# Gated attention and two MLPs on one core: two heads in column halves of the array, compact values and states, seven w_out slots, another order of the front

## The reference

```python
for t in range(S):
    state = f[:, :, t, :, None] * state + np.einsum('bhd,bhe->bhde', k[:, :, t], v[:, :, t])
    y[:, :, t] = np.einsum('bhd,bhde->bhe', q[:, :, t], state)
```

## Time and profile before

| | us |
|---|---|
| runs of the kernel | 919.07, 920.27, 920.87 (median 920.27) |
| the profiled execution | 919.11 |
| its span, first to last instruction | 917.4 |
| front, to the first `up` | 61.7 |
| attention steps beside `up` | 61.7 to 358 |
| PE busy over the span | 857.0 (93%) |
| DVE, ACT, POOL busy | 486.3, 373.7, 227.9 |

### The profile page before, as it was taken

One profiled execution on the slowest core, in us unless ns is written; L12 is line 12 of the kernel. 1 busy time (PEld: TensorE's weight loads), 2 busy tenths in 40 slices (PEclk: granted clock), 3 DMA queues, 4 the chain that ended last, 5 costly groups with the idle time before them and its releaser, 6 DMA issues.

```text
span 917.4 us, 16237 instructions
## 1 busy us (share of the span) xinstructions
PE 857.0 (93%) x6097; PEld 769.5 (84%) x6097; DVE 486.3 (53%) x1269; ACT 373.7 (41%) x826; POOL 227.9 (25%) x226
## 2 busy tenths in 40 slices
PE   4769999999999999999999999999877999999994
PEld 3548888888888888888888888889777999999994
DVE  7347656666666653546677877777612222222120
ACT  5345555445545543533223333322223444444431
POOL 5800000000001000120000000000015677777741
PEclk9879999999999999999999999999997999999998
DMA  9735444444455434554544543434402555555510
GB/s 232 209 81 140 119 136 138 130 121 136 133 139 137 130 100 146 195 189 121 150 138 127 155 128 116 129 90 128 155 36 81 161 169 148 165 159 184 166 50 26
DMA packets 80214, 123.66 MB, mean 135 GB/s; under 512 B 32912, under 2 KB 57488, under 8 KB 80144
## 3 DMA queue, kind: packets, MB, share of 16 engines
q1 hardware_dynamic: 65488, 75.23, 30.1%
q0 software_dynamic: 10560, 42.48, 13.1%
q10 hardware_dynamic: 4096, 5.02, 2.3%
HBM read 83.37 MB, written 34.60 MB: 129 GB/s over the span
## 4 chain that ended last, share of the span: by engine, by line
PE 84%; DVE 10%; DMA 2%; issue 1%; ACT 1%; POOL 1%; SPq 0%; ACTq 0%; POOLq 0%; DVEq 0%
PE ps_h L1375 14%; PE ps_h L1377 13%; PE ps_h L1376 13%; PE ps_y L1348 5%; PE ps_heads L1321 4%; PE ps_heads L1375 4%; PE ps_heads L1376 3%; PE ps_heads L1377 3%; PE ps_gate L1417 3%; PE ps_k L1484 3%; PE ps_gate L1375 2%; PE ps_u L1375 2%; PE ps_k L1328 2%; PE ps_gate L1377 2%; PE ps_gate L1376 2%; PE ps_u L1377 2%
## 5 line engine op out<-in xcount | busy, mean ns | idle before, releaser
L1375 PE MATMUL ps_h<-x_hi,w_hi 128*128 128x384 f32 x576 | 206.3, 358 | 8.3 <-DVE x_lo L1041 7.1
L1377 PE MATMUL ps_h<-x_hi,w_lo 128*128 128x384 f32 x576 | 195.3, 339 | 0.0
L1376 PE MATMUL ps_h<-x_lo,w_hi 128*128 128x384 f32 x576 | 194.8, 338 | 0.0
L874 ACT ACTIVATE g_hi<-qk 128x384 fp32r<-128x384 f32 x128 | 67.1, 525 | 176.1 <-PE ps_h L1377 95.4
L1046 DVE TENSOR_TENSOR w_raw<-ps_h,w_raw 128x384 f32<-128x384 f32 x128 | 71.2, 556 | 122.3 <-ACT w_raw L845 121.9
L1375 PEld LDWEIGHTS ps_h<-x_hi,w_hi 128*128 128x128 f32 x576 | 109.7, 190 | 16.8 <-issue 8.5
L682 POOL DMA_DIRECT2D g_kept<-w_raw x64 | 34.8, 544 | 338.8 <-DVE w_raw L1046 338.8
L1376 PEld LDWEIGHTS ps_h<-x_lo,w_hi 128*128 128x128 f32 x576 | 110.0, 191 | 0.0
L1377 PEld LDWEIGHTS ps_h<-x_hi,w_lo 128*128 128x128 f32 x576 | 109.5, 190 | 0.0
L732 POOL TENSOR_TENSOR w_lo<-w_raw,w_hi 128x1536 fp32r<-128x1536 f32 x28 | 97.9, 3512 | 40.6 <-ACT w_hi L918 40.5
L845 ACT ACTIVATE w_raw<-ps_h 128x384 f32<-128x384 f32 x128 | 62.4, 488 | 95.7 <-PE ps_h L1377 95.4
(11 more groups left out here) (202 smaller groups left out, 1714.0 us busy)
## 6 DMA issues: line engine op xcount, KB each, us to landing
g_kept<-w_raw POOLq DMA_DIRECT2D x64, 384.0 KB, 2.9
qk<-g_kept SPq DMA_DIRECT2D x64, 384.0 KB, 3.3
w_raw<-w SPq DMA_DIRECT2D x32, 768.0 KB, 4.5
qk<-qkf SPq DMA_DIRECT2D x64, 144.0 KB, 3.4
vals<-v SPq DMA_DIRECT2D x64, 72.0 KB, 3.9
x_rows<-cum_rel POOLq DMA_DIRECT2D x24, 192.0 KB, 4.1
qk<-qkf SPq DMA_DIRECT2D x60, 72.0 KB, 2.2
w_raw<-w_in POOLq DMA_DIRECT2D x4, 768.0 KB, 7.7
```

Of the source, the lines that this page charges most:

```text
L874: nc.scalar.activation(g_hi[:, n % GB, :], g_raw[:, slot, n % 2 * BLK:(n % 2 + 1) * BLK], ACT.Copy)\
L1375: nc.tensor.matmul(to, a_hi, b_hi, start=start, stop=False)
L1376: nc.tensor.matmul(to, a_hi, b_lo, start=False, stop=False)
L1377: last = nc.tensor.matmul(to, a_lo, b_hi, start=False, stop=stop)
```

## The change

Values are kept 96 wide, without the zeros, and loaded with one DMA for each pair and block instead of two. The state of each head is 48 columns wide in its own 48 partitions, so the mask goes and L1014 becomes a multiplication with one scalar. The update, y and the state's part of y become two matmuls each, one for each head, whose 48 columns lie in column half 0 or 64 of the array; for the state the 48 rows lie in row half 0 or 64 too. y now stands in partitions 0 to 47 and 64 to 111, and `ship` sends each head by itself: 2, 3, 3 and 2 DMAs for the four pairs instead of 1, 2, 2 and 1. Two memsets of PSUM replace those of the mask and of the values.

In the front there are seven slots for w_out, and SP issues all 16 tiles before the gates, keys and values of block 1. Turn-outs begin at step 4, the last two and the last `gate_out` follow the last step. The gates of pairs 2 and 3 are worked one to two steps earlier. Behind the last step the cumulation of pair 4 comes ahead of the first split; `factors` and `scale` of pair 5 move behind `up` 0, and `turn_gates` behind `up` 1. Block 1's steps take slots 1 to 12, later blocks start one slot later. The first load of w_in waits for gates instead of keys.

```diff
@@ -45,7 +45,7 @@
 HP = 64 + HD
-PV = 3 * HD
+PV = 2 * HD
 PACE = 14
...
@@ -65,11 +65,11 @@
 GATE_LAG = 2
-WIN = 4
+WIN = 7
 OUT_SLOT = 102
-AHEAD = 2
+AHEAD = 1
 TURN_SLOTS = 5
-TURNS = {3: 1, 4: 1, 5: 2, 6: 2, 7: 2, 8: 2, 9: 2, 10: 2, 11: 2}
+TURNS = {4: 1, 5: 1, 6: 2, 7: 2, 8: 2, 9: 2, 10: 2, 11: 2}
 FIRST_PIECE = 40
...
@@ -101,8 +101,8 @@
         k_rows = sb("k_rows", [P, 2, HP])
-        state = sb("state", [HP, PAIRS, 2, 2 * HD])
-        state_sum = sb("state_sum", [HP, PAIRS, 2 * HD])
+        state = sb("state", [HP, PAIRS, 2, HD])
+        state_sum = sb("state_sum", [HP, PAIRS, HD])
         y_pair = sb("y_pair", [P, PAIRS, BLK])
...
@@ -197,8 +196,8 @@
         turn_row_banks = [ps_heads[:, 0, :], ps_k[:], ps_y[:]]
-        y_area = ps_y[0:2 * HD, 0:P]
-        update_area = ps_u[0:HP, 0:2 * HD]
+        y_area = ps_y[0:HP, 0:P]
+        update_area = ps_u[0:HP, 0:HD]
         key_area = ps_k[:, 0:HP]
...
@@ -357,8 +355,8 @@
                 yield "logs", m
-            beside = {1: [("cumulate", 2)], 2: [("factors", 2)], 3: [("cumulate", 3), ("scale", 2)],
-                      4: [("factors", 3)], 5: [("scale", 3)]}
+            beside = {0: [("cumulate", 2)], 1: [("factors", 2), ("cumulate", 3)], 2: [("scale", 2), ("factors", 3)],
+                      3: [("scale", 3)]}
             f = 0
...
@@ -372,19 +370,19 @@
             yield from settle(STEPS - 1)
+            while f < FT:
+                yield "turn_out", f
+                f += 1
+            yield "gate_out", FT // 4 - 1
             yield "logs", 4
+            yield "cumulate", 4
+            yield "split", 0, 0
+            yield "split", 0, 1
             yield "logs", 5
-            yield "gate_out", FT // 4 - 1
-            yield "turn_gates", 0
-            yield "split", 0, 0
-            yield "cumulate", 4
-            yield "split", 0, 1
             yield "cumulate", 5
+            yield "split", 0, 2
             yield "factors", 4
-            yield "split", 0, 2
             yield "scale", 4
-            yield "factors", 5
-            yield "scale", 5
...
@@ -393,7 +391,7 @@
                 t, i = divmod(n, STEPS)
-                at.setdefault(i if t == 1 else (t - 1) * PACE - AHEAD + i * PACE // STEPS, []).append(n)
+                at.setdefault(i + 1 if t == 1 else (t - 1) * PACE - AHEAD + i * PACE // STEPS, []).append(n)
             first = {n // (2 * CB): slot for slot, ns in at.items() for n in ns if n % (2 * CB) == 0}
...
@@ -407,6 +405,11 @@
                 yield "up", t, j
+                if slot == 0:
+                    yield "factors", 5
+                    yield "scale", 5
+                if slot == 1:
+                    yield "turn_gates", 0
                 if slot >= GATE_LAG and (slot - GATE_LAG) % 4 == 3:
...
@@ -541,10 +544,9 @@
                 t, hp = divmod(m, PAIRS)
-                vsrc = v[t // 2 * PAIRS + hp].rearrange("p (c h d) -> p c h d", c=CH, h=2)
-                vdst = vals[:, hp].rearrange("p c (h d) -> p c h d", d=HD)
-                for h in range(2):
-                    sp.dma_start(vdst[:, :, 2 * h], vsrc[:, t % 2 * CB:(t % 2 + 1) * CB, h]).then_inc(v_in[hp], 16)
+                at = t % 2 * CB * PV
+                sp.dma_start(vals[:, hp].rearrange("p c n -> p (c n)"), v[t // 2 * PAIRS + hp][:, at:at + CB * PV])\
+                    .then_inc(v_in[hp], 16)
...
@@ -559,22 +561,19 @@
                 load_keys(m)
+            for m in (2, 3):
+                load_values(m)
             sp.wait_ge(gate_w_zeroed, 1)
             sp.dma_start(gate_w[:, :, 0:EXPERTS], w_gate.rearrange("(k p) e -> p k e", p=P)).then_inc(gate_in, 16)
-            load_out_tile(0)
-            load_values(2)
-            load_out_tile(1)
-            load_values(3)
-            for f in range(2, WIN):
+            for f in range(FT):
                 load_out_tile(f)
-            for m in range(PAIRS, 2 * PAIRS):
-                load_gates(m)
-            for what, *a in opening():
-                if what == "turn_out" and a[0] + WIN < FT:
-                    load_out_tile(a[0] + WIN)
-                elif what == "ship":
-                    load_keys(PAIRS + a[1])
-                    load_values(PAIRS + a[1])
+            for group in (range(PAIRS, PAIRS + 2), range(PAIRS + 2, 2 * PAIRS)):
+                for m in group:
+                    load_gates(m)
+                for m in group:
+                    load_keys(m)
+                for m in group:
+                    load_values(m)
             for m in range(2 * PAIRS, 3 * PAIRS):
...
@@ -652,15 +650,17 @@
                 .then_inc(consts, 1)
-            pool.wait_ge(consts, 6)
+            pool.wait_ge(consts, 5)
             nc.gpsimd.memset(qk[32:64, 2:4, 0:2], 0.0).then_inc(zeroed[1], 1)
                 _, src, tiles = weight_piece(g, 0)
-                if g < 2:
-                    pool.wait_ge(qk_in[g], 32)
+                if g == 0:
+                    pool.wait_ge(f_in[1], 32)
+                if g == 1:
+                    pool.wait_ge(qk_in[1], 32)
...
@@ -808,24 +808,26 @@
                     reached(act, xt_in[hp], 16 * ship_parts(hp) * t)
-                nc.scalar.activation(y_pair[0:2 * HD, hp, cb * P:(cb + 1) * P], y_area, ACT.Copy)\
+                nc.scalar.activation(y_pair[0:HP, hp, cb * P:(cb + 1) * P], y_area, ACT.Copy)\
                     .then_inc(y_copied, 1)
             def ship_parts(hp):
-                return 1 if hp in (0, PAIRS - 1) else 2
+                return 2 if hp in (0, PAIRS - 1) else 3
                 reached(act, x_lo_ready, (t - 1) * KT)
-                row = hp * 2 * HD
-                done = 0
-                while done < 2 * HD:
-                    k, p = divmod(row + done, P)
-                    n = min(P - p, 2 * HD - done)
-                    act.dma_start(xT[p:p + n, t % 2, k, :], y_pair[done:done + n, hp, :]).then_inc(xt_in[hp], 16)
-                    done += n
+                for h in range(2):
+                    row = (2 * hp + h) * HD
+                    done = 0
+                    while done < HD:
+                        k, p = divmod(row + done, P)
+                        n = min(P - p, HD - done)
+                        act.dma_start(xT[p:p + n, t % 2, k, :], y_pair[64 * h + done:64 * h + done + n, hp, :])\
+                            .then_inc(xt_in[hp], 16)
+                        done += n
...
@@ -964,17 +966,15 @@
             nc.vector.memset(qk[32:64, 0:2, 0:2], 0.0).then_inc(zeroed[0], 1)
-            nc.vector.memset(pair_mask[:], 0.0).then_inc(mask_zeroed, 1)
-            dve.wait_ge(mask_zeroed, 1)
-            for h in range(2):
-                nc.vector.memset(pair_mask[64 * h:64 * h + HD, h * HD:(h + 1) * HD], 1.0).then_inc(consts, 1)
+            nc.vector.memset(ps_u[0:HP, 0:HD], 0.0).then_inc(consts, 1)
+            nc.vector.memset(ps_y[0:HP, 0:P], 0.0).then_inc(consts, 1)
                 if m == 0:
-                    dve.wait_ge(consts, 6)
+                    dve.wait_ge(consts, 5)
                 nc.vector.tensor_tensor_scan(cum, restart[:], log_f[0:HP, m % 2, :], 0.0, ALU.mult, ALU.add)\
...
@@ -1011,9 +1011,8 @@
                 c = t % 2 * CB + cb
-                nc.vector.scalar_tensor_tensor(out=state[:, hp, before % 2, :], in0=src,
-                                               scalar=step_f[:, hp, factor:factor + 1], in1=pair_mask[:],
-                                               op0=ALU.mult, op1=ALU.mult).then_inc(state_ready, 1)
+                nc.vector.tensor_scalar(state[:, hp, before % 2, :], src, step_f[:, hp, factor:factor + 1], None, ALU.mult)\
+                    .then_inc(state_ready, 1)
...
@@ -1331,26 +1330,29 @@
                 if cb == 0:
-                    pe.wait_ge(v_in[hp], 32 * (t + 1))
+                    pe.wait_ge(v_in[hp], 16 * (t + 1))
                 if has_keys(n):
                         pe.wait_ge(*update_read[kb - 1])
-                    both_heads = vals[:, hp, cb, :].rearrange("p (h d) -> p h d", d=HD)[:, 0:3:2, :]
-                    nc.tensor.matmul(update_area, k_rows[:, kb % 2, :], both_heads, start=True, stop=True)\
-                        .then_inc(update_done, 1)
+                    for h in range(2):
+                        last = nc.tensor.matmul(update_area[64 * h:64 * h + HD, :], k_rows[:, kb % 2, 64 * h:64 * h + HD],
+                                                vals[:, hp, cb, h * HD:(h + 1) * HD], start=True, stop=True)
+                    last.then_inc(update_done, 1)
                 pe.wait_ge(scores_masked, n + 1)
                 for h in range(2):
-                    last = nc.tensor.matmul(y_area, vals[:, hp, cb, h * HD:h * HD + 2 * HD],
-                                            scores[:, n % 2, h], start=h == 0, stop=c == 0 and h == 1)
+                    last = nc.tensor.matmul(y_area[64 * h:64 * h + HD, :], vals[:, hp, cb, h * HD:(h + 1) * HD],
```

(12 more changed lines are left out.)

## The result

The changed kernel takes 932.65 us (median of 4 runs, 932.5 to 932.71) against 919.67 us before (4 runs, 915.7 to 920.87): 1.0149 times as long, interval 1.0117 to 1.018, slower by 13 us. The forecast was 921.2 with a range to 931. The profiled execution has a span of 930.9 us (before 917.4).

A forecast was written before the change was run, and what follows sets the result against it. PE was taken to bound the kernel behind the front, and to wait only in the front. Front -10.0, steps +9.1, `turn_gates` +1.7 and block 1's x +0.7 sum to +1.5 us; forecast 921.2 us, range 911 to 931.

The forecast's parts named there:

- The step: Attention steps in slots: transpose to `up` streaming takes 1.13 to 1.14 us instead of 1.00; 84 steps cost +9.1 us.
- Rival C: Steps in slots: changes of array division cost less than those seen, say half; 909 us, faster; chance 0.13.
- B: Rival: the state's two half products write one PSUM bank and run one after the other; +15.7 us, 937; chance 0.10.
- `turn_gates`: Between `up` 1 and the first score: PE waits for `leak` and the copy, then turns the gates; +1.7 us.
- the ship's additional DMA: Slots: one more DMA, 32 times, 0.55 to 0.6 us of ACT each, hidden by PE's work; uncovered 18 us.
- +0.7 (0 to 2.5): Block 1's x: shipping one slot later and one DMA more, partly won back, cost 0.7 us.
- a wait of under 2.5 us before block 1: Sign to look for: PE waits less than 2.5 us before block 1's first `up`.
- the front's "-10.0": Front: `up` 0 starts at 52 us (51 to 53) instead of 61.72, 10.0 us gained; bounds -5 and -14.
- clock, worth 2: Front: fewer pauses on PE avoid time at the lower clock, gaining 2 us.
- w_out's wait: Front: 4.4 us of PE's idle time come from late w_out tiles and go with seven slots.
- if all goes well: Front: the last y's copy ends at 43.5 us in the good case, about 44.3 otherwise.
- less idle keeps the clock: Front: with less idle time on PE the clock stays up, worth 2 us.

The follow-up runs named there:

- e1: Kernel before with only the column halves, compact values and states, and per-head ships; old front, slots and four w_out slots: 930.29 us, ratio 1.0138.
- e3: Kernel before with the new front, whole-array matmuls and four w_out slots, attention steps in their old slots: 911.63 us, ratio 0.991.
- e4: Changed kernel with the later attention steps put back in their old slots: 925.05 us, ratio 1.0062.
- e5: e2 with only the ship of y changed, issued by head, 10 DMAs a block instead of 6: 918.62 us, ratio 1.0003.
- e14: Changed kernel with the gates' work of each block's last slot but one put behind the next slot's split of x: 930.59 us, ratio 1.0133.
- e6: Changed kernel with 20 matmuls of 128x128 zeros on PE ahead of the first score: 928.46 us, ratio 1.0117.
- e9: e6 with two more matmuls of zeros in each of the front's twelve steps: 938.88 us.
- e2: Kernel before with the new front and steps one slot later, but whole-array matmuls and four w_out slots: 911.23 us, ratio 0.9918.
- e8: Kernel before with halves for update and values, but the state as one block-diagonal 112x112 matmul ahead of the update; old front and slots: 929.42 us, ratio 1.0126.
- e13: e8 with the update too as one whole-array 112x96 matmul, masked on DVE, so only the values' matmuls stay in halves: 940.03 us, ratio 1.0225.
- e7: e3 with 20 matmuls of 128x128 zeros on PE ahead of the first score: 909.74 us, ratio 0.9908.
- e11: e7 with one more matmul of zeros in each of the front's twelve steps: 911.52 us.
- e10: Changed kernel with four w_out slots instead of seven: 932.43 us.
- e12: Changed kernel with the gates' work of pairs 8 and on started one slot earlier: 934.73 us.

## Why the prediction was wrong

**The step was right.** 1.15 us measured for 1.13 to 1.14, 0.095 at each change of division in the rows, y's pairs 0.007 us apart. e1's blocks are 9.3 us longer. Without the longer waits before blocks 3 and 6 (1.25), and with 2.0 us less at half clock in block 0 put back (1.0), that is 9.0 for 9.1 forecast. (The forecast's terms as written add up to 9.3; with 12 x 0.01 for its 0.2 they give 9.1.) Rival C is out. So is B, whose 937 is the rivals' number nearest to the 932.65 measured. The state's two products write one bank from different row halves and start 0.007 us apart, so what the Trainium skill says ("TensorEngine Tiling (Array Packing)", Gotcha 1: PSUM Pressure), that different row tiles can't access the same bank simultaneously, doesn't hold back this pair, whose partitions of the bank are disjoint too: all 80 such pairs of the trace start 0.006 or 0.007 us apart.

**`turn_gates` was right.** 1.1 us of wait (forecast 1.2), and block 0 in e3 is 1.1 longer than before with 1.3 us less of it at 1.2 GHz, so 1.8 for 1.7.

**The step that failed first: the ship's additional DMA "in slots ... is hidden by PE's own work", and "+0.7 (0 to 2.5)" for block 1.** It looked at the slack of one landing and at nothing else that stands in ACT's order ahead of x_hi. PE waits 2.31 us before block 1, 2.03 before block 3 and 0.51 before block 4, and no longer 0.53 before block 6: 4.0 more than before. Two waits inside blocks are new, 0.4 for scores in block 1 and 0.9 for `leaky` in block 4. Behind the two long waits 10.2 us run at half clock; e4's blocks 1 and 3, without a fall, are 1.5 and 3.0 us shorter once the waits are taken out, so 4.5 are lost. That is 9.8 where 0.7 stood. The sum behind `up` 0 then is 9.0 + 1.8 + 9.8, less 0.4 for less half clock in block 0: 20.2, measured 19.9. The prediction's own sign, a wait of under 2.5 us before block 1, came true; its price for that wait, and the clock behind it, did not.

e5 shows the cause of block 3's wait without any halves, e14 that ACT's queue makes half of it. Block 1's is a landing (x_hi waited 2.64 us for the transfer), and its cause is open: it was 2.06 to 2.46 us in the four kernels with halves and shift but no warm matmuls, 0.40 and 0.42 in the two with them (e6, e9), and 0.30 and 0.41 in e2 and e5.

**The step that failed second: the front's "-10.0", of it "clock, worth 2".** w_out's wait went, as forecast, and PE's idle time between first step and last y fell from 7.8 to 0.7 us, more than the 6 forecast. But the last y ended at 46.6 instead of 44, because the rise of the clock moved from 19 to 36 us: 24.5 us of the steps run at 1.2 GHz, 15.1 before. The tail behind took 8.9 for 8.5. The prediction's own terms give less than its 10.0, too: 44.3 and 8.5 are 52.8, 8.9 before 61.72, and even the 43.5 of "if all goes well" gives 9.7. The new front by itself gave 9.2 (e3) and 12.2 (e2), so the forecast of it was right for whole-array matmuls. It was the halves, and what goes with them, that spent it: e4's `up` 0 is 6.8 later than e3's and the changed kernel's 6.1 later than e2's, while 12 steps at 0.14 are 1.7. The prediction took "less idle keeps the clock" for granted; the changed front has less idle and less clock.

**Why the sum missed.** Both failures are meetings of two parts: e1 adds 10.5, e3 takes 8.1, sum +2.4, near the forecast of +1.5; together (e4) they are +5.3; with the shift, which alone costs nothing, +13. The last step, 7.6 us, is clear of the noise. The 2.9 between +2.4 and +5.3 is not: e1 and e3 alone are known to 3 us each. There only the start of `up` 0 speaks for a meeting. The range held none of this, as it added independent bounds. Its chances are off by a little as well: the parts named for "slower" add up to 0.44, not 0.42.

**What stays open.** Why the clock rises later with the halves. More work doesn't bring the rise forward (e9), leaving out the state's halves doesn't either (e8, 33.2), and e13 lies between. The ships by head alone don't do it (e5, 22.5), but compact values beside whole matmuls were not tried. A kernel with halves in the slots only was not tried; neither was one in which block 1's landing is made early. And nothing here shows why the long matmuls of e8 and e13 are slower.

**The better version.** The new front with whole-array matmuls and four slots: e2, e3, e7 and e11 are 909.7 to 911.6 us, 0.991 to 0.992 of before, and faster than the changed kernel by 21 to 23 us. Warm matmuls add nothing that can be told from e3.

## What to carry to other kernels

Halving the columns of short matmuls buys streaming time and pays a gap of 0.095 us at every change of division, and the first weights in the open: count the changes before the columns. When each PE stage begins with an operand from an in-order engine, list all that its queue issues in the slot ahead, DMA issues included, and price a new wait with the clock that may fall behind it. Two edits that are each harmless may meet in one slot: time them alone and together.

## What was not expected of the hardware

- With column halves in its steps, a TensorE that was busy for 23.2 of 24.0 us (11 to 35 us) stayed at its lower speed, while before, busy for 19.9 of the same 24.0, it rose at 19 us. Whole-array matmuls put between (e9) made the slow time longer.
- Waits of 1.0 to 1.6 us before block 3 left the clock alone six times (e1, e2, e4, e8, e13, e14); each of 2.03 to 2.46 before blocks 1 and 3 (the changed kernel, e5, e6, e9, e10, e12, e14) came with 3.4 us or more at 1.2 GHz. But in e13 one of 2.12 before block 6 left it alone, and in e12 one of 1.99 did, while one of 1.49 before block 4 and one of 1.15 inside block 1 came with 3.4 us each. The length of the wait alone doesn't tell whether the clock falls.
- Between kernels that are the same up to `up` 0, it moved by 3 us and more with the rise of the clock (e2 16.6 and 49.5, e3 25.4 and 52.5; the changed kernel 36.0 and 55.6, e4 44.2 and 59.3).
- Two kernels (e8, e13) ran all their long matmuls 1 to 2% slower (0.176 us from start to start instead of 0.174), at the same granted clock.
